# Gates written to DRAM and gathered per block, GpSimd's loop written out, and an entry of the second expert stage by high parts first

## What is computed

```python
x = attention(q, k, v, n_global, n_local)      # 4 batches, 8 heads, 768 positions, 64 wide -> x (3072, 512)
# first mixture: 8 experts, 512 -> 1024 -> 512, one expert per token
logits = x @ w_gate
e_idx = np.argmax(logits, axis=1)
gate_w = softmax(logits)[np.arange(N), e_idx]
eom = 1.0 / (1.0 + np.exp(-(x @ w_output_gate)))
for e in range(E):
    mask = e_idx == e
    ye = np.maximum(x[mask] @ w1[e], 0.0) @ w2[e]
    out[mask] = gate_w[mask, None] * eom[mask, e, None] * ye
# second mixture: tokens are assigned in the order of all logits, at most 384 per expert
assigned = greedy(x2 @ w2_gate, cap=N // E)
out[assigned == e] = np.maximum(x2[assigned == e] @ w21[e], 0.0) @ w22[e]
```

## Time and profile before

| | us |
|---|---|
| three runs | 1042.23, 1039.45, 1041.18 |
| median | 1041.18 |
| the profiled execution, its own time | 1038.73 |
| its span from the first to the last instruction | 1036.6 |
| TensorE busy in the span | 913.8 (88%) |
| VectorE busy | 679.4 (66%) |
| ScalarE busy | 451.5 (44%) |
| GpSimd busy | 187.7 (18%) |
| mean granted TensorE clock, share of full speed | 0.925 |

### The profile page before, as it was taken

How to read it: one execution, slowest core, us unless ns; L and a number is a source line. 1 busy time by engine, 2 the same in 40 slices (tenths; PEclk the granted TensorE clock), 3 DMA queues, 4 the chain that set the end, 5 groups by cost and what they waited for, 6 DMA issues and landing times.

```text
span 1036.6 us, 22299 instructions
## 1 busy us (share of the span) xinstructions
PE 913.8 (88%) x6398; PEld 768.6 (74%) x6399; DVE 679.4 (66%) x1824; ACT 451.5 (44%) x983; POOL 187.7 (18%) x246
## 2 busy tenths in 40 slices
PE   6888999994899999999999995444699999999994
PEld 3777777773688888888888883333499899989993
DVE  5677888768766968869777786555454645364511
ACT  3678888856434352535525251000143434343410
POOL 2122232300211111111111120000203312331211
PEclk9899999997999999999999996555699999999997
DMA  9567777452351524515334342000226353635100
GB/s 213 105 153 161 164 167 164 105 194 83 115 202 48 205 74 169 201 52 201 123 121 135 123 153 96 1 2 2 61 86 222 125 200 123 221 123 201 40 31 31
DMA packets 146569, 129.43 MB, mean 125 GB/s; under 512 B 102464, under 2 KB 114752, under 8 KB 146368
## 3 DMA queue, kind: packets, MB, share of 16 engines
q1 hardware_dynamic: 137696, 99.68, 32.5%
q0 software_dynamic: 8800, 28.84, 8.3%
HBM read 107.79 MB, written 20.71 MB: 124 GB/s over the span
## 4 chain that ended last, share of the span: by engine, by line
PE 71%; DVE 9%; issue 6%; SPq 5%; DMA 3%; ACT 2%; DVEq 2%; ACTq 0%; POOL 0%; POOLq 0%
PE ps_s L1300 14%; PE ps_o L1323 14%; PE ps_o L1698 9%; PE ps_s L1682 6%; PE ps_pT L1682 6%; PE ps_s L1698 4%; PE ps_t L1859 3%; DMA qn<-in_q 3%; PE ps_pT L1311 2%; PE ps_o L517 2%; SPq L2112 2%; DVE product L1529 1%; SPq L2131 1%; PE ps_s L487 1%; PE ps_pT L500 1%
## 5 line engine op out<-in xcount | busy, mean ns | idle before, releaser
L1323 PE MATMUL ps_o<-w_split_parts,hs 128*128 x696 | 166.6, 395 | 1.0 <-ACT hs L1410 0.5
L1300 PE MATMUL ps_s<-w_split_parts,xs 128*128 x696 | 165.5, 393 | 0.9 <-ACT xs L1402 0.9
L1529 DVE SCALAR_TENSOR_TENSOR product<-y_sb,wg_all 128x512 bf16<-128x512 f32 x224 | 145.8, 688 | 7.6 <-issue 2.1
L1323 PEld LDWEIGHTS ps_o<-w_split_parts,hs 128*128 128x128 f32 x696 | 128.5, 188 | 27.9 <-issue 1.7
L1300 PEld LDWEIGHTS ps_s<-w_split_parts,xs 128*128 128x128 f32 x696 | 128.5, 188 | 26.5 <-issue 1.2
L833 ACT ACTIVATE arena_p<-arena_p,min_s 128x256 f32<-128x256 f32 (+1 forms) x192 | 92.3, 484 | 27.7 <-DVE min_s L698 27.1
L1698 PE MATMUL ps_o<-w_split_parts,hs 128*128 128x512 f32 x384 | 94.1, 397 | 0.0
L1520 DVE TENSOR_TENSOR w_split_parts<-raw,w_split_parts 128x1024 f32 (+1 forms) x68 | 78.8, 1221 | 19.7 <-ACT w_split_parts L1421 18.3
L1698 PEld LDWEIGHTS ps_o<-w_split_parts,hs 128*128 128x128 f32 x384 | 70.2, 188 | 15.9 <-ACT hs L1732 2.9
L1410 ACT ACTIVATE hs<-ps_pT 128x512 fp32r<-128x512 f32 x58 | 31.6, 596 | 113.6 <-PE ps_pT L1311 109.5
L1778 DVE TENSOR_TENSOR w_split_parts<-raw,w_split_parts 128x1024 fp32r<-128x1024 f32 x56 | 68.6, 1225 | 17.6 <-ACT w_split_parts L1740 17.4
(11 more groups left out here) (321 smaller groups left out, 1661.8 us busy)
## 6 DMA issues: line engine op xcount, KB each, us to landing
raw<-in_moe_w SPq DMA_DIRECT2D x32, 2048.0 KB, 9.2
y_rows<-y_sb POOLq DMA_DIRECT2D x31, 256.0 KB, 2.4
kn<-in_k SPq DMA_DIRECT2D x32, 192.0 KB, 3.5
qn<-in_q SPq DMA_DIRECT2D x32, 192.0 KB, 3.6
vn<-in_v SPq DMA_DIRECT2D x32, 192.0 KB, 2.9
x_rows<-arena_x SPq DMA_DIRECT2D x96, 64.0 KB, 1.6
va<-in_v SPq DMA_DIRECT2D x32, 120.0 KB, 2.7
wg_rows<-in_moe_w_gate SPq DMA_DIRECT2D x1, 2048.0 KB, 7.8
```

Of the source, the lines that this page charges most:

```text
L1300: last = nc.tensor.matmul(ps_s[:, f, :], xs[:, a, c * P:(c + 1) * P], weights(par, w, cols), start=(n == 0), stop=(n == len(passes) - 1))
L1323: last = nc.tensor.matmul(ps_o[:, bank, :], hs[:, a, c * P:(c + 1) * P], weights(par, 2 + w, slice(c * DM, (c + 1) * DM)), start=(n == 0), ...
L1529: nc.vector.scalar_tensor_tensor(product[:, e % 2, :], y_sb[:], 1.0, wg_all[:, e, :], ALU.mult, ALU.mult, accum_out=log_now[:, e:e + 1])
```

## The change

The gates no longer go through a table. DVE stops at the gates themselves, TensorE turns them once (24 rows of 128), ScalarE copies them to SBUF and writes them to a DRAM tensor of one number per token, and GpSimd gathers 128 of them per block with the same row numbers as x. GpSimd's three loops of the first expert stage are written out block by block, so that each gather takes its row numbers from `rows_i` at a fixed column, with no copy. In the second expert stage GpSimd's first gathers use `rows2_i` itself and wait for the second count of `tables` only; `up` waits for the high parts, and for the low parts only before the first product that uses them; and eight matmuls without use are put between the first transposes.

```diff
@@ pe_experts
+            pe.wait_ge(gate_made, 1)
+            nc.tensor.transpose(ps_s[0:TILES, 2, 0:P], gate[:, 0:TILES], ident[:]).then_inc(gate_turned, 1)
             turn_x(0)
             up(0)
             turn_x(1)
-            pe_table(pe, ps_o[:, 1, :], len(chunks(TILES)), TILES, 3, BLK1)
             turn_h(0)
@@ dve_routing1 (dve_gate_table and dve_gates are gone too)
-            done(nc.vector.tensor_tensor(gate[:, 0:C], t2[:, 0:C], m_open[:, 0:C], ALU.mult))
-            for part in range(3):
-                done(nc.vector.tensor_copy(gate_parts[:, part, 0:C], gate[:, 0:C]))
-                if part < 2:
-                    done(nc.vector.tensor_tensor(gate[:, 0:C], gate[:, 0:C], gate_parts[:, part, 0:C], ALU.subtract))
+            nc.vector.tensor_tensor(gate[:, 0:C], t2[:, 0:C], m_open[:, 0:C], ALU.mult).then_inc(gate_made, 1)
@@ act_gates
+            act.wait_ge(gate_turned, 1)
+            nc.scalar.activation(gate_rows, ps_s[0:TILES, 2, 0:P], ACT.Copy).then_inc(gate_copied, 1)
+            act.wait_ge(gate_copied, 1)
+            act.dma_start(gate_dram.rearrange("(c p) o -> c (p o)", p=P), gate_rows).then_inc(gate_stored, 16)
@@ act_experts
             def scale_y(b):
+                act.wait_ge(gate_in, b * 16 + 16)
...
-            act.wait_ge(gates_known, 1)
             begin(0)
+            act.wait_ge(gate_stored, 16)
@@ pool_experts
+            def gather_gate(b):
+                if b == 0:
+                    pool.wait_ge(gate_stored, 16)
+                else:
+                    pool.wait_ge(gate_in, b * 16)
+                nc.gpsimd.indirect_dma_start(out=gates[:, b:b + 1], out_offset=None, in_=gate_dram[:, :],
+                                             in_offset=bass.IndirectOffsetOnAxis(rows_i[:, b:b + 1], 0),
...
+            for b in range(BLK1 + 3):
+                if b < BLK1:
+                    gather(b)
+                if 1 <= b < BLK1 + 1:
+                    gather_gate(b - 1)
+                if b >= 3:
+                    put(b - 3)
@@ pe_experts2, up
-                pe.wait_ge(rows2_low, e * CB + CB)
+                if half == 0:
+                    pe.wait_ge(rows2_high, e * CB + CB)
...
+                        if f == 0 and a == 1 and c == 0:
+                            pe.wait_ge(rows2_low, e * CB + CB)
@@ pe_experts2
+            pe.wait_ge(tables, 3)
             for j in range(CB):
                 turn_rows(0, j)
+                keep_busy((5, 0, 3)[j], ps_s[:, 2, :])
@@ pool_experts2
+            pool.wait_ge(tables, 2)
+            gather(0)
             pool.wait_ge(tables, 3)
-            gather(0)
```

More of the change, by code:

```diff
@@ L60, in program @@
     y_dram = nc.dram_tensor("y_rows", (BLK1 * P, DM), f32).ap()
+    gate_dram = nc.dram_tensor("gate_rows", (NT, 1), f32).ap()
     q_p, k_p, v_p = [t.rearrange("b (g a) (i r) d -> (b g) a r i d", a=2, r=P) for t in (q, k, v)]
@@ L294, in program @@
         blocks_known = sem("blocks_known")
-        gates_known = sem("gates_known")
+        gate_made = sem("gate_made")
+        gate_turned = sem("gate_turned")
+        gate_copied = sem("gate_copied")
+        gate_stored = sem("gate_stored")
+        gate_in = sem("gate_in")
         slow_tables = sem("slow_tables")
@@ L1215, in dve_routing1 @@
             done(nc.vector.reciprocal(m_open[:, 0:C], m_open[:, 0:C]))
-            done(nc.vector.tensor_tensor(gate[:, 0:C], t2[:, 0:C], m_open[:, 0:C], ALU.mult))
-            for part in range(3):
-                done(nc.vector.tensor_copy(gate_parts[:, part, 0:C], gate[:, 0:C]))
-                if part < 2:
-                    done(nc.vector.tensor_tensor(gate[:, 0:C], gate[:, 0:C], gate_parts[:, part, 0:C], ALU.subtract))
-        def dve_gate_table(dve):
-            for part in chunks(TILES):
-                dve_vals(part, 3, BLK1, gate_parts).then_inc(row_hots, 1)
-        def dve_gates(dve):
-            dve.wait_ge(tabled, 2)
-            high, mid, low = [ps_o[:, 1, part * BLK1:(part + 1) * BLK1] for part in range(3)]
-            nc.vector.tensor_copy(gates[:], low)
-            dve.drain()
-            nc.vector.tensor_tensor(gates[:], gates[:], mid, ALU.add)
-            dve.drain()
-            nc.vector.tensor_tensor(gates[:], gates[:], high, ALU.add).then_inc(gates_known, 1)
+            nc.vector.tensor_tensor(gate[:, 0:C], t2[:, 0:C], m_open[:, 0:C], ALU.mult).then_inc(gate_made, 1)
         def act_routing1(act):
@@ L1794, in gather @@
             def gather(e):
-                if not isinstance(e, int) or e > 0:
+                rows = rows2_i
+                if not is_first(e):
                     for j in range(CB):
                         pool.wait_ge(rows2_in[j], e * 16)
-                nc.gpsimd.tensor_copy(rows2_now[:], rows2_i[:, bass.ds(e * CB, CB)]).then_inc(rows2_copied, 1)
-                pool.wait_ge(rows2_copied, e + 1)
+                    rows = rows2_now
+                    nc.gpsimd.tensor_copy(rows2_now[:], rows2_i[:, bass.ds(e * CB, CB)]).then_inc(rows2_copied, 1)
+                    pool.wait_ge(rows2_copied, e)
                 for j in range(CB):
-                    if not isinstance(e, int) or e > 0:
+                    if not is_first(e):
                         pool.wait_ge(rows2_turned, e * CB + (j + 1 - CB))
```

38 lines of the change are left out of this document (12 added, 26 removed).

## The result

The changed kernel takes **1032.81 us** (median of 8 runs, 1031.15 to 1036.04) beside 1041.09 us for the kernel before (8 runs on the same chip, 1037.44 to 1044.42). The ratio is **0.9926**, 95% interval 0.9906 to 0.9945: 7.7 us less, between 5.7 and 9.8. The forecast was 1040.1 us within 1037.0 to 1043.4, most likely no measurable change.

The account below looks back on a forecast made before the run. TensorE was taken to bound both expert loops, leaving room only at their entries: 0.2 us at the first plus 0.9 at the second, 1.1 us off the 1041.18 us median, so 1040.1 us, range 1037.0 to 1043.4.

Parts of the forecast that it names:

- Room is left only at the two entries: Both expert stages' loops: TensorE is fed (busy 322.49 of 323 us in the first), so only their entries can gain.
- Cost nothing: First stage's loop: one gate gather per block, about 1.02 us of GpSimd issue each, hidden, so no cost.
- stays through an idle microsecond: Second entry: full clock, granted from 741.4, survives idle time; the eight added matmuls cost at worst 0.2 us.
- The rival that spoke of the clock: First entry: TensorE's clock halves in its new pauses, third gather issued 5.8 us later, 1045.9 us in all; chance 0.13.
- The second entry: Second expert stage's start: earlier gathers 0.27 us plus `up` not awaiting low parts 0.63, gain 0.9 us (bounds 0 and 1.1).
- Rival B: First entry stays flat and second gives nothing, TensorE's idle time being its own sequencer: 1041.0 us; chance 0.08.
- The first entry: First expert stage up to `down_(0)`: table hidden behind the third gather's landing; gain 0.2 us (gain 2.7 to loss 2.9).
- at the same moment: First entry: third gather issued at 274.2 as now, the dropped 1.13 us copy paying for 1.15 us added.
- rival A: First entry: third gather lands early, table was the real cost; gain there 2.7, in all 3.6 us, 1037.5; chance 0.19.
- Rival C: First entry: TensorE's clock falls to half in new pauses, `up(0)` takes 11.5 us for 5.76; 1045.9 us; chance 0.13.
- Rival D: First entry: ScalarE's DMA issue takes 1.5 to 3.5 us, not 0.4; sum 1041 to 1043.2 us; chance 0.05.
- the sign of being wrong that the prediction named: First stage's loop: ScalarE waiting for GpSimd's gates, which the prediction put at nothing.

Follow-up runs that it names:

- e5: e4 plus 31 small GpSimd gathers that nothing reads, spread over the first stage's blocks: 1031.64 us, ratio 0.9920 to the kernel before.
- e6: e4 plus 5 small GpSimd gathers that nothing reads, in the first stage's blocks: one run of 1031.59 us.
- e10: e4 plus five small direct GpSimd DMAs that nothing reads, in place of the five gathers of e6: one run of 1032.68 us.
- e4: Kernel before with GpSimd's loops written out and the second entry changed, gate table kept, no gate gathers: 1036.02 us, ratio 0.9962.
- e13: Kernel before plus only five small direct GpSimd DMAs without use, behind the first stage's last store: 1034.71 us, ratio 0.9950.
- e1: The kernel before, unchanged, measured again: 1039.46 us, ratio 0.9998.
- e2: Kernel before with only GpSimd's loops written out and no row copy, gate table kept: 1040.86 us, ratio 1.0014.
- e11: Kernel before with only the 5 and 3 matmuls without use at the second entry, and a wait ahead of them: 1037.89 us, ratio 0.9978.
- e3: Kernel before with everything the change does at the second expert stage's entry and nothing else: 1037.58 us, ratio 0.9986.
- e8: Changed kernel plus 24 matmuls without use where the gate table's stood: 1030.93 us, ratio 0.9925 to the kernel before.
- e12: Changed kernel without the 5 and 3 matmuls without use at the second entry: 1033.62 us, ratio 0.9940 to the kernel before.
- e14: Changed kernel plus four matmuls without use where the gate table's stood: 1032.69 us, ratio 0.9929 to the kernel before.
- e17: The changed kernel measured again, on one chip with e18: 1032.47 us, ratio 0.9940 to the kernel before.
- e9: e4 plus one small GpSimd gather that nothing reads, in the last of the first stage's gathering blocks: one run of 1036.28 us.
- e18: e10 measured again, on one chip with e17: 1032.45 us, ratio 0.9937 to the kernel before.

## Why the prediction was wrong

**The step that failed** is the first: "Room is left only at the two entries." It was read from the windows of the two loops; what lies behind the last matmul was not read. There are 13.88 us of before's span, of which GpSimd's DRAIN takes 9.06. The gates' gathers were priced as issues ("Cost nothing") when they were 31 DMAs more on an engine whose end-of-program work goes by their number. That is 4.57 us, and all rivals' sums were without it. e5, e6 and e10 show it against e4, without the gates' way, and e13 with no other part of the change at all.

**The second term missing** is the clock. The prediction read "stays through an idle microsecond" from one profile and gave the eight added matmuls a cost of at most 0.2 us and no gain. In that profile the clock had held; in e1's and e2's of the same entry it hadn't. e11 puts the matmuls alone at 2.3 us (0.5 to 4.1), against the kernel before over many executions; the two profiles of before and after, both at 1.00, hold none of it. The rival that spoke of the clock looked at the first entry, and for a loss.

**The third** goes the other way: TensorE's branch in the loop, 1.8 us (346.25 against 344.4), which fits code that moved and which no term of the sum had.

**The second entry was right in mechanism, and came out smaller.** The forecast was 0.9 us, with 8.9 us from the finished row numbers to `up`. Counted like that, from the end of DVE's 0.18 us, the two profiles give 9.79 and 9.14: 0.65. (The table counts from its start, 9.97 and 9.32; there the 14 other profiles with the new entry, all but before, after, e1, e2, e11 and e13, have 8.81 to 9.70.) Rival B, the entry giving nothing, is out as far as `up` goes: with the matmuls alone (e11) the distance stays at 9.83, with the waits changed too (e3) it is 9.31, so TensorE did wait for DVE's low parts. But not all of it reaches the end of the stage. Adding the stage behind, it is 285.71 us in before and 285.58 in after, 0.1 less; over all profiles in which the clock held, the three with the old entry have a mean of 285.9 and the fourteen with the new one 285.4, 0.5 less.

**The first entry was right in mechanism, and its 0.2 us is within what varies.** Forecast and trace, counted from the gates: TensorE's `up(0)` would come 1.15 us later than before, and came 1.43 later (264.96 - 262.42 = 2.54 against 265.77 - 264.66 = 1.11), in the main because ScalarE's DMA issue took 0.59 and not 0.4 us; `up(1)` stood behind another 1.00 us of "issue" that the sum didn't have, in which TensorE's queue loads the block's buffer number and expert; the third gather would be issued "at the same moment", and was (9.60 and 9.54 us behind the gates); it would take 7.2 us to land and took 7.9; TensorE would stand idle 1.7 us ahead of `turn_x(2)` and stood 1.14.

`down_(0)` itself hangs on the landing, as the prediction had it: it came 1.7 us behind it both before and now (281.57 less 272.02 + 7.9; forecast 1.74). In before, TensorE's queue took up the loads behind `turn_x(2)` just when the gather had landed (274.20 + 7.4 = 281.6), although TensorE itself came to these transposes only at 282.23. One row of its queue (ns, then where in the span), one of TensorE:

```profile
L1272 PEldq TENSOR_LOAD <-blk_par x1: 307/307/307, 281.7 to 281.7; - x1
282.23 0.60 PE L1286 MATMUL ps_t<-ident,xg 128*128 128x128 f32 x4
```

So rival A's early landing did not come in this profile, and the table's 4.24 us went into waiting for the landing. In e8, e12 and e14 TensorE does not wait ahead of `turn_x(2)`, and `down_(0)` stands 35.4 to 35.5 us behind the ranks, against 36.5 and 36.6 in after and e17. Rival A it is not: where the landing is on record (e14) it took 6.7 us from 271.85, so it came at 278.5, just as `up(1)` ended, and `down_(0)` followed it by 1.7 us again:

```profile
278.55 0.66 PE L1274 MATMUL ps_t<-ident,xg 128*128 128x128 f32 x4
280.24 5.04 PE L1311 MATMUL ps_o<-w_split_parts,hs 128*128 x21 [1.04 <-issue]
```

Over the five profiles with the gates' way the mean is 35.9, over the fifteen with the table 36.5 (35.6 to 37.5; 36.9 and more in e13 and in the five where the clock fell near 273, e2, e3, e4, e9 and e18): a gain of 0.6 at most, not 2.7, and without those five profiles 0.2. The Trainium skill ("DMA: Bandwidth & Descriptors", Queues, rings and completion order) has each DMA engine change queue after a packet; the early landing that the prediction worked out from this isn't borne out by the 7.9 us here, beside a median of 4.0 for all 31 gathers of this line:

```profile
DMA to landing us min/median/max: 3.3/4.0/8.3
```

Rival C (the clock falling in TensorE's new pauses at the first entry) did not happen: none of the five profiles with the gates' way shows it. Rival D is out (0.59 us). The gathers of gates are hidden from TensorE, as forecast: GpSimd is busy 82.44 of 323 us in the loop (forecast 77), and TensorE waits for none of them. But the sign of being wrong that the prediction named, ScalarE waiting for them, is there: ahead of `scale_y` ScalarE waits for gates 7 times (engine, line, waited for: us in total, times, longest):

```profile
ACT y_sb L1418 <- DMA gates<-gate_rows,rows_i: 16.8, 7, 2.7
ACT y_sb L1418 <- DVE logits L1524: 16.1, 7, 2.5
```

```profile
ACT y_sb L1428 <- DVE logits L1534: 32.0, 14, 2.7
```

The last row is before: 14 waits there too, 32.0 us for 32.9 now. A wait is put down to what came last, so the gates' gathers took the place of waits for DVE and added at most 0.9 us in all, on an engine that does not bound the loop.

**The sum as measured:** 4.57 (DRAIN) + 2.3 (clock) + 0.1 to 0.5 (second entry) - 0.5 to + 0.6 (first) - 1.8 (branch) = 4.7 to 6.2 us, and the clock's term alone may be 1.8 us more or less. The timed difference is 7.7 (5.7 to 9.8) in the first comparison and 6.2 (4.2 to 8.4) in e17's. They agree within their intervals; what the other 1.5 to 3 us of the first are, if they are not noise, is open.

The ratios of the kernels in a row: written out 1.0014, second entry 0.9986, both 0.9962, both with 31 idle DMAs 0.9920, the change 0.9926. The step to the idle DMAs is the DRAIN's; the one from the first two to "both" is larger than any profile explains.

Not tried: the gates' way with GpSimd's loops kept, since a gather whose destination depends on a loop's counter would be needed there.
